# Expert layers of an attention and mixture-of-experts kernel: seven products in a run, then six tiles

## The reference, cut to what matters

```python
# attention: B=4, heads 8, S=576, D=64, with a learned bias; its output becomes
x = attn_out.transpose(0, 2, 1, 3).reshape(2304, 512)
logits = x @ w_gate                       # 8 experts
P = np.exp(logits - logits.max())
for _ in range(8):                        # balancing steps
    P /= P.sum(1, keepdims=True) + 1e-09
    P /= P.sum(0, keepdims=True) + 1e-09
    P *= N / E
for e in range(8):
    h = np.maximum(x @ w1[e], 0.0)        # 512 -> 1024
    out += P[:, e:e+1] * (h @ w2[e])      # 1024 -> 512
```

## Time and profile before

| | |
|---|---|
| median of 3 runs | 1875.35 us (1874.04 to 1876.37) |
| the profiled execution | 1875.39 us, of which the span is 1873.5 us |
| PE busy | 1853.5 us (99%) |
| PEld busy | 1600.3 us (85%) |
| DVE busy | 978.9 us (52%) |
| ACT busy | 759.6 us (41%) |
| POOL busy | 1076.4 us (57%) |

### The profile page before, as it was taken

How to read it: one execution, slowest core, us unless ns; L and a number is a source line. 1 busy time by engine, 2 the same in 40 slices (tenths; PEclk the granted TensorE clock), 3 DMA queues, 4 the chain that set the end, 5 groups by cost and what they waited for, 6 DMA issues and landing times.

```text
span 1873.5 us, 27898 instructions
## 1 busy us (share of the span) xinstructions
PE 1853.5 (99%) x10255; PEld 1600.3 (85%) x10255; DVE 978.9 (52%) x1846; ACT 759.6 (41%) x1314; POOL 1076.4 (57%) x720
## 2 busy tenths in 40 slices
PE   8999999999999999999999999999999999999999
PEld 4677776688999999998999999999989999999998
DVE  8877777757543444346434443444464434443443
ACT  8776777532333333334333333333333333333332
POOL 0223225456766666666676666666666666666662
PEclk9999999999999999999999999999999999999999
DMA  7763451111111111112111111111121112111110
GB/s 243 220 150 90 127 148 41 52 54 60 68 68 68 68 68 68 68 68 102 68 68 68 68 68 68 68 68 68 68 102 68 68 68 68 68 68 68 68 68 34
DMA packets 44160, 152.55 MB, mean 81 GB/s; under 512 B 9594, under 2 KB 18042, under 8 KB 29710
## 3 DMA queue, kind: packets, MB, share of 16 engines
q1 hardware_dynamic: 44046, 151.04, 24.9%
HBM read 135.69 MB, written 15.34 MB: 81 GB/s over the span
## 4 chain that ended last, share of the span: by engine, by line
PE 94%; DVE 2%; issue 0%; ACT 0%; DVEq 0%
PE banks L646 14%; PE banks L645 14%; PE banks L644 14%; PE banks L612 12%; PE banks L614 12%; PE banks L616 12%; PE banks L525 5%; PE banks L486 4%; PE banks L468 3%; PE banks L469 2%; PE banks L551 1%; PE banks L496 0%; DVE h_lo L1114 0%; DVE probs L978 0%; DVE x_lo_first L1021 0%
## 5 line engine op out<-in xcount | busy, mean ns | idle before, releaser
L1222 POOL TENSOR_TENSOR w_lo<-stage,w_hi 128x1024 fp32r<-128x1024 f32 (+1 forms) x288 | 639.8, 2222 | 521.7 <-ACT w_hi L801 514.8
L646 PE MATMUL banks<-w_hi,h_lo 128*128 128x512 f32 x1152 | 455.1, 395 | 0.0
L645 PE MATMUL banks<-w_lo,h_hi 128*128 128x512 f32 x1152 | 453.8, 394 | 0.0
L612 PE MATMUL banks<-x_hi,w_hi 128*128 128x384 f32 x1344 | 452.4, 337 | 0.0
L616 PE MATMUL banks<-x_hi,w_lo 128*128 128x384 f32 x1344 | 451.5, 336 | 0.0
L644 PE MATMUL banks<-w_hi,h_hi 128*128 128x512 f32 x1152 | 448.0, 389 | 1.2 <-DVE h_lo L1114 1.2
L844 ACT ACTIVATE h_hi<-corner 128x384 fp32r<-128x384 f32 x288 | 149.7, 520 | 539.6 <-DVE corner L1107 539.6
L1107 DVE TENSOR_TENSOR corner<-u,banks 128x384 f32<-128x384 f32 x288 | 159.2, 553 | 387.0 <-PE banks L616 386.5
L801 ACT ACTIVATE w_hi<-stage 128x1024 fp32r<-128x1024 f32 (+1 forms) x288 | 282.2, 980 | 1.5 <-PE banks L525 1.5
L612 PEld LDWEIGHTS banks<-x_hi,w_hi 128*128 128x128 f32 x1344 | 252.5, 188 | 16.8 <-issue 1.2
L614 PE MATMUL banks<-x_lo_rest,w_hi 128*128 128x384 f32 x768 | 257.8, 336 | 0.0
(11 more groups left out here) (102 smaller groups left out, 2084.3 us busy)
## 6 DMA issues: line engine op xcount, KB each, us to landing
stage<-in_expert_w SPq DMA_DIRECT2D x96, 1024.0 KB, 4.7
raw<-in_qk SPq DMA_DIRECT2D x32, 576.0 KB, 7.1
bias_scratch<-bias_out SPq DMA_DIRECT2D x36, 288.0 KB, 2.6
bias<-bias_scratch SPq DMA_DIRECT2D x16, 288.0 KB, 2.8
v_main<-in_v SPq DMA_DIRECT2D x16, 256.0 KB, 2.7
bias<-bias_scratch SPq DMA_DIRECT2D x16, 256.0 KB, 3.7
out<-total SPq DMA_DIRECT2D x4, 768.0 KB, 4.3
out<-total SPq DMA_DIRECT2D x6, 256.0 KB, 2.0
```

Of the source, the lines that this page charges most:

```text
L612: pe.matmul(dst, hi[:, w, f], x_hi[:, k, c, :], start=fresh and c == 0, stop=False, skip_group_check=not fresh)
L645: pe.matmul(dst, h_hi[:, g % 2, f, tokens], lo[:, f], start=False, stop=False)
L646: mm = pe.matmul(dst, h_lo[:, g % 2, f, tokens], hi[:, f], start=False, stop=fp == FPAIRS - 1 and f == 1)
L1222: pool.tensor_tensor(lo, of, hi.bitcast(F32), ALU.subtract).then_inc(w_split, 1)
```

## The change

- PE takes all seven products and then all six tiles (`TOGETHER`). Only in the first period of the second and third pair (g = 32 and 64) the former interleaving stays (`APART`). Before, the interleaving stood in every period.
- ACT copies product 2 into a fourth slot of `corner` (`keep_corner`); product 4 waits for that copy, and rounding and splitting of the first block read the copy.
- The small matmuls of the balancing steps stand behind tiles, each behind a wait for the period's fourth `combined`; the next period's product 0 waits until DVE has read them.
- ACT: the rounding of the first weight part stands behind the first hidden block; input parts 1 and 3 are rounded later.
- DVE: the five combines come first, with only the first hidden split between the third and fourth; then the other splits, balancing steps and adds. Input parts 2 and 3 are split in the next pair's first period, parts 4 to 6 stand between u3 and the first corner.

```diff
-TILES_AFTER = ((), (0, 1), (), (2, 3), (), (4,), (5,))
+APART = ((), (0, 1), (), (2, 3), (), (4,), (5,))
+TOGETHER = ((), (), (), (), (), (), tuple(range(TJ)))
-        TOTALS = [(3 + i // 2, 1 + 3 * (i % 2)) for i in range(ITERS)]
-        TOP_ROW = (1, 4)
-        TOP_ALL = (2, 1)
+        TOP_ROW = (1, 2)
+        TOP_ALL = (1, 5)
+        TOTALS = [(2, 4), (3, 0), (3, 4), (5, 0), (5, 4), (6, 0), (6, 4), (7, 0)]
+        def tiles_after(g, k):
+            return (APART if 0 < g < ALL and g % PERIODS == 0 else TOGETHER)[k]
@@ PE, product
+                    if g - 1 == TOP_ALL[0]:
+                        pe.wait_ge(top_neg, 1)
+                    if TOTALS[0][0] < g <= TOTALS[-1][0] + 1:
+                        pe.wait_ge(totals_kept, sum(t[0] < g for t in TOTALS))
                 elif k == 4:
-                    pe.wait_ge(h_split, 4 * g + 1)
+                    pe.wait_ge(corner_kept, g + 1)
@@ PE, after each tile
+            def side_work(g, j):
+                if (g, j) not in [TOP_ROW, TOP_ALL] + TOTALS:
+                    return
+                pe.wait_ge(combined, 5 * g + 4)
...
@@ ACT
+            def keep_corner(g):
+                act.wait_ge(product_done, NP * g + 3)
+                if g > 0:
+                    act.wait_ge(h_split, 4 * g - 3)
+                act.activation(corner[:, 0, :], product_bank(g, 0), ACT.Copy).then_inc(corner_kept, 1)
@@ DVE, one period after the change
+                if at == 0 and p > 0:
+                    split_factor(p, 2)
                 dve.wait_ge(product_done, NP * g + 2)
                 dve.wait_ge(p1_kept, g + 1)
                 combine(u2[:], product_bank(g, 1), p1_copy[:], ALU.add)
+                if at == 0 and p > 0:
+                    split_factor(p, 3)
+                dve.wait_ge(product_done, NP * g + 4)
+                combine(u3[:], product_bank(g, 1), p1_copy[:], ALU.add)
                 if at == 0 and p > 0:
                     for k in range(4, NP):
                         split_factor(p, k)
+                dve.wait_ge(product_done, NP * g + 5)
+                dve.wait_ge(combined, 5 * g + 2)
+                combine(corner[:, 1, :], product_bank(g, 0), u3[:], ALU.add)
...
                 split_hidden(g, 0)
+                if after:
+                    split_factor(p + 1, 0)
+                dve.wait_ge(product_done, NP * g + 6)
+                combine(corner[:, 2, :], product_bank(g, 1), u3[:], ALU.subtract)
+                dve.wait_ge(product_done, NP * g + 7)
+                combine(corner[:, 3, :], product_bank(g, 0), u2[:], ALU.add)
+                split_hidden(g, 1)
                 if g == 2:
                     sinkhorn_rows(0)
+                read_side(g, 0)
+                add_tile(g - 1, 0)
+                split_hidden(g, 2)
+                read_side(g, 2)
+                add_tile(g - 1, 1)
+                split_hidden(g, 3)
+                add_tile(g - 1, 2)
                 if after:
                     split_factor(p + 1, 1)
+                for j in range(3, TJ):
+                    read_side(g, j)
+                    add_tile(g - 1, j)
```

More of the change, by code:

```diff
@@ L165, in bass_attention_moe @@
         h_hi = sb("h_hi", [P, 2, 2, 2 * T], F32R)
-        corner = sb("corner", [P, 3, T])
+        corner = sb("corner", [P, 4, T])
         h_lo = sb("h_lo", [P, 2, 2, 2 * T], F32R)
@@ L209, in bass_attention_moe @@
         h_rounded = sem("h_rounded")
+        corner_kept = sem("corner_kept")
+        totals_kept = sem("totals_kept")
         h_split = sem("h_split")
@@ L289, in product_bank, with side @@
             return banks[:, (g + which) % 2, 0:T]
-        def side(g, k):
-            return (g + PRODUCTS[k][1]) % 2
+        def side(g):
+            return banks[:, (g + 1) % 2, SIDE:SIDE + P]
+        def tiles_after(g, k):
+            return (APART if 0 < g < ALL and g % PERIODS == 0 else TOGETHER)[k]
         def x_low(k):
@@ L676, in turn_logits, with turn_top, spread_top, column_totals @@
                 mm.then_inc(logit_turned, 1)
-            def turn_top():
+            def turn_top(g):
                 pe.wait_ge(top_ready, 1)
-                pe.transpose(banks[0:1, side(*TOP_ROW), SIDE:SIDE + P], top[:, 0:1], ident[:]).then_inc(top_turned, 1)
-            def spread_top():
+                pe.transpose(side(g)[0:1, :], top[:, 0:1], ident[:]).then_inc(top_turned, 1)
+            def spread_top(g):
                 pe.wait_ge(top_found, 2)
                 pe.wait_ge(ones_set, 1)
-                pe.matmul(banks[:, side(*TOP_ALL), SIDE:SIDE + 1], ones[0:1, :], top_row[0:1, 1:2], start=True,
-                          stop=True).then_inc(top_all, 1)
-            def column_totals(k):
+                pe.matmul(side(g)[:, 0:1], ones[0:1, :], top_row[0:1, 1:2], start=True, stop=True).then_inc(top_all, 1)
+            def column_totals(g, k):
                 pe.wait_ge(col_ready, k + 1)
-                pe.matmul(banks[:, side(*TOTALS[k]), SIDE:SIDE + E], ones[:], col_part[:], start=True,
-                          stop=True).then_inc(col_all, 1)
+                pe.matmul(side(g)[:, 0:E], ones[:], col_part[:], start=True, stop=True).then_inc(col_all, 1)
+            def side_work(g, j):
+                if (g, j) not in [TOP_ROW, TOP_ALL] + TOTALS:
+                    return
+                pe.wait_ge(combined, 5 * g + 4)
+                if (g, j) == TOP_ROW:
+                    turn_top(g)
+                elif (g, j) == TOP_ALL:
+                    spread_top(g)
+                else:
+                    column_totals(g, TOTALS.index((g, j)))
             for g in range(ALL + 1):
@@ L702, in _ @@
                     if g > 0:
-                        for j in TILES_AFTER[k]:
+                        for j in tiles_after(g, k):
                             second_layer(g - 1, j)
+                            side_work(g, j)
                 if g == 0:
@@ L836, in round_hidden @@
                 if i == 0:
-                    act.wait_ge(product_done, NP * g + 3)
+                    act.wait_ge(corner_kept, g + 1)
                     if g > 1:
                         act.wait_ge(h_used, g - 1)
-                    source = product_bank(g, 0)
                 else:
                     act.wait_ge(combined, 5 * g + 2 + i)
-                    source = corner[:, i - 1, :]
-                act.activation(h_block(h_hi, g, f, part), source, ACT.Relu).then_inc(h_rounded, 1)
+                act.activation(h_block(h_hi, g, f, part), corner[:, i, :], ACT.Relu).then_inc(h_rounded, 1)
+            def keep_corner(g):
[3 more added lines that the diff above has]
+                act.activation(corner[:, 0, :], product_bank(g, 0), ACT.Copy).then_inc(corner_kept, 1)
             def keep_logits():
@@ L871, in _ @@
                 keep_first(g)
[L872 to L875, removed]
                 if at == 0 and p > 0:
@@ L878, in _ @@
                         round_factor(p, k)
+                keep_corner(g)
+                if g == 1:
+                    place_logits()
                 round_hidden(g, 0)
+                if more:
+                    round_weights(g + 1, 0)
                 if g == 2:
@@ L882, in _ @@
                     act.activation(routing[:], routing[:], ACT.Exp, bias=top[:, 1:2]).then_inc(exp_ready, 1)
+                if after:
+                    round_factor(p + 1, 0)
                 if more:
                     round_weights(g + 1, 1)
+                round_hidden(g, 1)
                 if after:
-                    round_factor(p + 1, 0)
                     round_factor(p + 1, 1)
-                round_hidden(g, 1)
                 if more:
                     round_weights(g + 1, 2)
+                round_hidden(g, 2)
+                round_hidden(g, 3)
                 if after:
                     round_factor(p + 1, 2)
-                round_hidden(g, 2)
-                if after:
                     round_factor(p + 1, 3)
-                round_hidden(g, 3)
         @block.vector
@@ L1048, in largest_of_all @@
                 dve.wait_ge(top_turned, 1)
-                dve.tensor_reduce(top_row[0:1, 0:1], banks[0:1, side(*TOP_ROW), SIDE:SIDE + P], AX_X, ALU.max).then_inc(top_found, 1)
+                dve.tensor_reduce(top_row[0:1, 0:1], side(TOP_ROW[0])[0:1, :], AX_X, ALU.max).then_inc(top_found, 1)
                 dve.wait_ge(top_found, 1)
@@ L1054, in keep_top @@
                 dve.wait_ge(top_all, 1)
-                dve.tensor_copy(top[:, 1:2], banks[:, side(*TOP_ALL), SIDE:SIDE + 1]).then_inc(top_neg, 1)
+                dve.tensor_copy(top[:, 1:2], side(TOP_ALL[0])[:, 0:1]).then_inc(top_neg, 1)
             def over_experts(ap):
@@ L1072, in keep_totals @@
                 dve.wait_ge(col_all, k + 1)
-                link(dve.tensor_scalar(col_sum[:], banks[:, side(*TOTALS[k]), SIDE:SIDE + E], EPS, None, ALU.add))
+                dve.tensor_scalar(col_sum[:], side(TOTALS[k][0])[:, 0:E], EPS, None, ALU.add).then_inc(totals_kept, 1)
```

(23 more changed lines are left out.)

9 lines of the change are left out of this document (removed).

## The result

The changed kernel takes 1879.20 us (median of 13 runs, 1877.53 to 1882.69) against 1874.96 us of the kernel before (13 runs). The ratio is 1.0026 with a 95% interval of 1.0017 to 1.0034: slower by 4.2 us. The forecast was 1879.5.

A forecast was written before the change was run, and what follows sets the result against it. PE was taken to bound the kernel, busy 480.00 of 480.00 us in the expert part. Terms -12.5 + 10.3 + 2.8 + 3.5 - 0.06 were summed to +4.1 on 1875.39, giving 1879.5 us, range 1868 to 1887.

The forecast's parts named there:

- Order on PE: In 93 expert periods, one change each way between products and tiles saves 0.135 us per period: -12.5 us.
- Handovers: Product k+2 directly one product behind k: combines on time cost 0, with some 0.06 us of room; at worst +14 us.
- rival E: Handovers between products slip 0.05 us each, three per period: +14 us, 1893 us in all; chance 0.10.
- Ordinary periods: DVE, ACT and POOL finish splits, adds and weights before PE needs them in ordinary periods: cost 0.
- Boundaries: Last period of a pair and first of the next: late DVE splits and adds cost 5.2 us, twice: +10.3.
- Clock: Behind the two 4.0 us PE gaps, a 3.4 us stretch at 1.2 GHz each: +2.8 us (0 to 3.4).
- Rival B: The clock holds: no half-clock stretch follows the boundary gaps, so 1876.7 us; chance 0.22.
- Balancing steps: First expert periods: new PE waits around balancing steps and scalings, 8 us instead of 4.3, less 0.25: +3.5 (1 to 8).
- Rival C: DVE's backlog at boundaries and balancing steps meets POOL idle: short splits, input parts on time, no half clock, 1867 us; chance 0.18.

The follow-up runs named there:

- 2: As 1, but from period 8 on, except periods 31, 63 and 95, products and tiles are interleaved with the former DVE order; 1873.64 us.
- 3: As 1, but in 44 periods the tiles stand in two groups of three, behind products 5 and 6; 1867.06 us in one run.
- 4: As 1, but from period 8 on DVE makes one or two one-column copies before u3 in periods with g % 4 = 1 or 2; 1863.68 us.
- 8: As 1, but from period 8 on DVE makes three or four one-column copies before u3 in periods with g % 4 = 1 or 2; 1868.95 us.
- 5: The changed kernel without the six DVE adds of periods 32 and 64; 1869.32 us in one run.
- 6: The changed kernel, but in periods 32 and 64 POOL starts its third remainder and sums only after DVE's last hidden split; 1875.64 us in one run.
- 1: The changed kernel, but in periods 32 and 64 DVE works in the order of the kernel before; 1863.71 us, ratio 0.9944 to the kernel before.

## Why the prediction was right, step by step

- *Order on PE*, -12.5: right. 82 ordinary periods take 15.506 or 15.507 us, and 2 and 3 show that it is the changes of kind. The rule of the Trainium skill ("TensorE: Matmul & The Clock Gate", section "Back-to-back issue gap"), which the page gives for a matmul by itself, has no such term; this case's traces measure 0.067 us for a change there and back.
- *Handovers*, 0: right, and rival E had less ground than I gave it. My room of 0.06 us was too small; 4 and 8 measure 0.12.
- *Ordinary periods*: right, no wait, although DVE's 384 h_lo splits went from 0.81 us on average (0.91 for the three blocks read from `corner`, 0.56 for the one read from PSUM) to 1.71. Of them 371 are now held by POOL.
- *Boundaries*, +10.3 without the clock: the mechanism was right and the size short. Periods 32 and 33, 64 and 65 are 39.5 and 39.9 us, and against before, with the order's gain taken out, cost 15.3 with the clock where I had 13.1. PE's waits there add up to 11.1 us, over the 8 under which the prediction would have been wrong. Period 32 came as counted (17.70 us). The loss in 33 was 0.7 longer, 4.6 for the gap and 0.1 for the first matmuls behind it: I let the second split follow POOL's first sum, but POOL began its next sum at 874.89 and DVE the split at 874.91, so it was held once more. 0.02 us decided 0.6.
- *Clock*, +2.8: right in kind. What periods 33 and 65 take over 15.51, less 4.6 for the gap and 0.1 for the restart (as in 5, without low clock), is 1.6 and 2.0, 3.6 together. Rival B falls for these two gaps. My ground, that a longer gap than that of the earlier trace rows brings the same, was weaker than I took it: the changed kernel's own trace has that attention wait without low clock.
- *Balancing steps*, +3.5 with the 0.25 of period 0: measured by the periods 1 to 8, 6.65 us over 15.507 against 4.26 over 15.64, so +2.4, less 0.2 in period 0 (17.63 us against 17.82), so +2.2. It is the term that I had most wrong in proportion: PE loses 0.6, 0.2 and 0.9 us in front of product 3 of periods 6, 7 and 8, where I had 0.8, 1.3 (at product 0 of period 7) and 1.4.
- *Rival C* (DVE catches up when POOL is idle) did not come, and 6 shows that half of its condition would not have been enough: with POOL out of the way of the last splits the wait is 1.95 us, but the low clock still comes, period 32 still takes 17.68 us, and the time is 1875.64 and not 1867. Input parts that POOL does not hold were not tried. The time that C named, and less, came with DVE's other order (1).

The two errors, 2.2 us too little at the boundaries and about 1.3 too much in the balancing steps, have opposite signs, so the total is closer than its terms; that is luck. (The terms as printed add up to 4.0, not 4.1, which changes nothing.) The two profiled executions also differ in the attention part, which the change does not touch: period 1 starts at 367.55 instead of 369.87. That one execution has no low clock there, while the one before has two stretches of 3.4 us, one of them in the earlier trace rows; period 0 gives 0.2 of the difference. From period 1 on the changed kernel is 5.3 us longer by the traces, which is -12.4 + 15.3 + 2.4, and my terms for that part gave 4.3. The medians of the whole say 4.2. Why they say less than the traces is not shown, so the 0.3 us between forecast and median is closer than the working deserves.

## What to carry to other kernels

When an engine streams without a pause, look at the distances between its instructions by their place in the run: here two kinds of matmul mixed cost 0.2 us in 15.6, visible only against a long run of one kind. When work of a helping engine is put off to free an early slot, follow its list through the one period that differs from the others, here the boundary that kept the interleaved order: the splits and adds put behind the last corner cost PE 4.6 us there and nothing in the ordinary periods. A gap on PE can cost more than itself: behind the gaps of 2.3 us of 6 the low clock added another 1.5 in period 33.

## What the runs showed of the hardware

- In a long run at full clock, 384-column matmuls start 0.1733 us apart and 512-column ones 0.2267 (1.04 and 1.36 us for six). Behind a change of kind the first tile takes 0.029 more and the second 0.012, the first product behind two or more tiles 0.026, behind a single tile 0.004. Why was not tried.
- DVE's instructions with two inputs in SBUF are held by POOL's: in the changed kernel all 371 held splits of 384 columns end 0.41 or 0.42 us behind a POOL instruction, the held input parts of 768 columns 0.81 or 0.82, and a split that meets a remainder of 2.4 us at its start takes up to 2.75 where it takes 0.55 undisturbed. DVE's combines and adds, which read PSUM, are not held (0.53 to 0.56 us for all 480 combines, 0.73 to 0.75 for all 126 adds), and neither were the 96 splits of the kernel before that read PSUM (0.54 to 0.56).
- The granted clock fell to 0.5 behind the gaps of 4.77 us (for 3.4 and 6.8 us) and, in 6, behind those of 2.29 us (3.4 us, twice). It did not fall behind the gaps of 1.32 and 1.35 us in 5. The attention part's gap of 2.9 us had low clock at its end or behind it in nine of the ten profiled executions, and none in that of the changed kernel, so the length of a gap does not decide by itself; what else does was not tried.
